# Sliding-window attention in a fused attention and mixer kernel: scores of both key tiles folded over each other in PSUM, and the turned block masked by VectorE

## The reference

```python
# 2 batches x 8 heads, seq 768, head_dim 64, n_sink 4, window 128
scores = scale * np.matmul(q, k.transpose(0, 1, 3, 2))
is_sink = pos[None, :] < int(n_sink)
rel = pos[:, None] - pos[None, :]
in_window = (rel >= 0) & (rel < int(window))
scores = np.where(is_sink | in_window, scores, -1000000000.0)
scores = scores - np.max(scores, axis=-1, keepdims=True)
a = np.exp(scores)
a = a / (np.sum(a, axis=-1, keepdims=True) + 1e-09)
return np.matmul(a, v)
```

## Time and profile before

| | us |
|---|---|
| median of 3 runs | 461.25 (458.89 to 461.72) |
| the profiled execution | 462.87 |
| its span | 461.1 |
| PE busy | 435.3 |
| DVE busy | 227.0 |
| ACT busy | 171.4 |
| POOL busy | 176.4 |

### The profile page before, as it was taken

How to read it: one execution, slowest core, us unless ns; L and a number is a source line. 1 busy time by engine, 2 the same in 40 slices (tenths; PEclk the granted TensorE clock), 3 DMA queues, 4 the chain that set the end, 5 groups by cost and what they waited for, 6 DMA issues and landing times.

```text
span 461.1 us, 7348 instructions
## 1 busy us (share of the span) xinstructions
PE 435.3 (94%) x2752; PEld 376.1 (82%) x2752; DVE 227.0 (49%) x435; ACT 171.4 (37%) x418; POOL 176.4 (38%) x122
## 2 busy tenths in 40 slices
PE   0699999999995999999999999999999999999997
PEld 0477777777774889999999997887887889999885
DVE  1568777777745799422233465615615403332222
ACT  2256665566532876322334103524323321111221
POOL 2298777543000008887765300000000165433442
PEclk9999999999997999999999999999999999999999
DMA  6444642431000002000400005000002000000222
GB/s 205 181 145 136 218 133 101 149 116 43 1 1 5 1 2 91 1 0 18 166 1 0 1 13 228 0 1 0 1 1 91 0 0 1 1 0 0 81 101 91
DMA packets 9442, 26.80 MB, mean 58 GB/s; under 512 B 1216, under 2 KB 2240, under 8 KB 9408
## 3 DMA queue, kind: packets, MB, share of 16 engines
q1 hardware_dynamic: 8064, 21.11, 13.2%
q0 software_dynamic: 1344, 5.24, 3.2%
HBM read 23.20 MB, written 3.15 MB: 57 GB/s over the span
## 4 chain that ended last, share of the span: by engine, by line
PE 92%; DVE 3%; DMA 2%; ACT 1%; issue 1%; POOL 0%; SPq 0%; ACTq 0%; DVEq 0%
PE ps L1060 22%; PE ps L1061 22%; PE ps L1062 22%; PE ps L1109 7%; PE ps L1081 6%; PE ps L1091 5%; PE ps L1075 3%; DMA lims_i<-in_window 2%; PE ps L1122 2%; PE ps L1116 2%; PE ps L1093 1%; DVE x2l L981 0%; DVE x L978 0%; ACT x2h L689 0%; POOL zl L470 0%
## 5 line engine op out<-in xcount | busy, mean ns | idle before, releaser
L527 ACT ACTIVATE probs<-ps,neg_max 128x288 f32<-128x288 f32 (+2 forms) x96 | 46.0, 495 | 52.5 <-DVE neg_max L782 52.5
L1060 PE MATMUL ps<-tok_hi,zl 128*128 128x384 f32 x192 | 64.2, 335 | 0.2 <-POOL zl L470 0.2
L1061 PE MATMUL ps<-tok_lo,zh 128*128 128x384 f32 x192 | 64.1, 334 | 0.0
L1062 PE MATMUL ps<-tok_hi,zh 128*128 128x384 f32 x192 | 64.1, 334 | 0.0
L470 POOL TENSOR_TENSOR zl<-cos_sb,zh 128x768 fp32r<-128x768 f32 x8 | 19.0, 2370 | 70.7 <-ACT zh L631 70.6
L955 DVE TENSOR_TENSOR x_t<-ps,x_t 128x768 f32<-128x768 f32 x16 | 15.3, 957 | 58.9 <-PE ps L1062 58.8
L782 DVE TENSOR_REDUCE neg_max<-ps 128x1 f32<-128x288 f32 (+2 forms) x96 | 36.3, 420 | 15.1 <-PE ps L1081 15.0
L1060 PEld LDWEIGHTS ps<-tok_hi,zl 128*128 128x128 f32 x192 | 36.0, 188 | 0.6 <-POOL zl L470 0.6
L1061 PEld LDWEIGHTS ps<-tok_lo,zh 128*128 128x128 f32 x192 | 36.0, 188 | 0.0
L1062 PEld LDWEIGHTS ps<-tok_hi,zh 128*128 128x128 f32 x192 | 36.0, 188 | 0.0
L1075 PE MATMUL ps<-bias,ident_b 128*128 128x288 bf16 (+2 forms) x96 | 19.2, 284 | 15.6 <-DVE k_lo L846 15.6
(11 more groups left out here) (142 smaller groups left out, 1064.2 us busy)
## 6 DMA issues: line engine op xcount, KB each, us to landing
tok_raw<-in_w_tok SPq DMA_DIRECT2D x6, 768.0 KB, 6.5
k_raw<-in_k_t SPq DMA_DIRECT2D x8, 448.0 KB, 4.2
q_raw<-in_q_t SPq DMA_DIRECT2D x8, 384.0 KB, 3.5
v_raw<-in_v_p SPq DMA_DIRECT2D x8, 384.0 KB, 3.0
out<-o_sb SPq DMA_DIRECT2D x12, 256.0 KB, 2.0
sp_raw<-in_w_sp SPq DMA_DIRECT2D x3, 768.0 KB, 6.3
in_raw<-in_moe_w_in POOLq DMA_DIRECT2D x1, 2048.0 KB, 8.4
th_raw<-in_moe_w_theta POOLq DMA_DIRECT2D x1, 1024.0 KB, 9.7
```

What stands on the lines that cost most here:

```text
L527: act.activation(probs[i % 2][:, 0:ncols(i), h], s_ps[i % 2][:, h, 0:ncols(i)], ACT.Exp, bias=neg_max[:, i % 2, h:h + 1], accum_out=sums[: ...
L1060: pe.matmul(dst, w_lo, m_hi, start=first, stop=False)
L1061: pe.matmul(dst, w_hi, m_lo, start=False, stop=False)
L1062: return pe.matmul(dst, w_hi, m_hi, start=False, stop=last)
```

## The change

- Keys: the layout in DRAM has the sinks behind every key tile but the last, so tile 1 also gets a product of 288 columns (tile before, sinks, own tile).
- Masks: no bias on the window parts. Instead DVE copies, under a lower triangle, the own tile's scores over those of the tile before (`copy_predicated`, both heads in one instruction, PSUM to PSUM). The folded block of 128 columns and the 32 sinks behind it are what maxima and exponentials read (160 columns). A bias remains for the sinks: two products of 32 columns on 64 rows for each head, issued behind the first part of the scores. For tile 0 the full bias remains, also behind the first part.
- Turning: one transpose for each head, and one for the sinks from tile 1 on, all in one bank, two banks in turn. DVE multiplies the turned block of both heads by two triangles into four blocks (`diagonal`, 512 elements), the factors for V of the own tile and the tile before. ACT copies the sinks' columns only, after DVE's product, as both read one bank.
- Order: on DVE `maxima(m + 2)` comes before `diagonal(m)`.
- Start: the limits are loaded by ACT's queue at once; DVE makes the triangles, then q_lo and k_lo, and only then waits for the limits and makes the three biases.
- ACT and DVE have pairs 2 to 5 written out.

```diff
-K_COLS = 2 * P + (TILES - 2) * STEP
+K_COLS = P + (TILES - 1) * STEP
+FOLD = P + SINKS
...
-        pt_ps = banks[2]
+        pt_ps = [banks[2][:, b, :] for b in range(2)]
...
             load_qk(0, 0)
-            sp.dma_start(lims_i[:, 0:2], n_sink.partition_broadcast(P)).then_inc(s_lims, 16)
-            sp.dma_start(lims_i[:, 2:4], window.partition_broadcast(P)).then_inc(s_lims, 16)
             load_v(0, 0)
...
             def copy_pt(m, i):
-                act.wait_ge(s_pt[0], m + 1)
-                act.activation(p_t[i % 2][0][:, 0:pt_cols(i, 0)], pt_ps[:, 0, 0:pt_cols(i, 0)], ACT.Copy).then_inc(s_ptc[0], 1)
+                act.wait_ge(s_pt, m + 1)
+                if i:
+                    act.wait_ge(s_ptd, diagonals(m // TILES, i))
+                cols = slice(WIN, WIN + P) if i else slice(0, WIN)
+                act.activation(p_t[i % 2][:, cols], pt_ps[i % 2][:, cols], ACT.Copy).then_inc(s_ptc, 1)
...
+            act.dma_start(lims_i[:, 0:2], n_sink.partition_broadcast(P)).then_inc(s_lims, 16)
+            act.dma_start(lims_i[:, 2:4], window.partition_broadcast(P)).then_inc(s_lims, 16)
             act.wait_ge(s_qk, 32)
             act.activation(q_hi[0][:, :], q_raw[:, :], ACT.Copy, scale=SCALE).then_inc(s_first, 1)
...
-            with act.Fori(1, PAIRS - 1) as n:
+            for n in range(1, PAIRS - 1):
...
+            dve.tensor_scalar(tri_r[:, :], col[:, :], line[:, 0:1], None, ALU.is_le).then_inc(s_mask, 1)
+            dve.tensor_scalar(tri_c[:, 1, :], col[:, :], line[:, 0:1], None, ALU.is_ge).then_inc(s_mask, 1)
+            dve.tensor_scalar(tri_c[:, 0, :], col[:, :], line[:, 0:1], None, ALU.is_lt).then_inc(s_mask, 1)
...
+            dve.wait_ge(s_first, 2)
+            dve.scalar_tensor_tensor(q_lo[0][:, :], q_raw[:, :], SCALE, q_hi[0][:, :].bitcast(F32), ALU.mult,
+                                     ALU.subtract).then_inc(s_first, 1)
+            dve.tensor_tensor(k_lo[0][:, :], k_raw[:, :], k_hi[0][:, :].bitcast(F32), ALU.subtract).then_inc(s_first, 1)
 
             dve.wait_ge(s_lims, 32)
...
             def maxima(m, i):
+                cols = slice(0, P)
+                if i:
+                    dve.wait_ge(s_sc, 2 * m + 2)
+                    dve.copy_predicated(s_ps[i % 2][:, :, 0:P], tri_r[:, :].bitcast(I32).unsqueeze(1).broadcast_to([P, 2, P]),
+                                        s_ps[i % 2][:, :, FOLD:FOLD + P]).then_inc(s_fold, 1)
+                    dve.wait_ge(s_fold, diagonals(m // TILES, i))
+                    cols = slice(0, FOLD)
                 for h in range(2):
                     dve.wait_ge(s_sc, 2 * m + h + 1)
-                    dve.tensor_reduce(neg_max[:, i % 2, h:h + 1], s_ps[i % 2][:, h, 0:ncols(i)], AX.X, ALU.max,
+                    dve.tensor_reduce(neg_max[:, i % 2, h:h + 1], s_ps[i % 2][:, h, cols], AX.X, ALU.max,
                                       negate=True).then_inc(s_max, 1)
+
+            def diagonal(m, i):
+                dve.wait_ge(s_pt, m + 1)
+                dve.tensor_tensor(p_d[i % 2][:, :, :, :],
+                                  pt_ps[i % 2][:, 0:2 * P].rearrange("p (h q) -> p h q", h=2).unsqueeze(1).broadcast_to([P, 2, 2, P]),
+                                  tri_c[:, :, :].unsqueeze(2).broadcast_to([P, 2, 2, P]), ALU.mult).then_inc(s_ptd, 1)
...
                 for i in range(TILES):
-                    copy_pt(m + i, i)
                     if i < TILES - 2:
                         maxima(m + i + 2, i + 2)
                     elif not last:
                         maxima(m + i + 2, i + 2 - TILES)
+                    if i:
+                        diagonal(m + i, i)
...
-                for h in range(2):
-                    pe.matmul(s_ps[i % 2][:, h, 0:ncols(i)], ident_b[:, :], BIAS[i][:, :], start=True, stop=False)
-
-                for q_part, k_part in ((q_lo[b], k_hi[b]), (q_hi[b], k_lo[b]), (q_hi[b], k_hi[b])):
+                for part, (q_part, k_part) in enumerate(((q_lo[b], k_hi[b]), (q_hi[b], k_lo[b]), (q_hi[b], k_hi[b]))):
                     for h in range(2):
                         rows = slice(h * HD, (h + 1) * HD)
...
+                        mm = pe.matmul(s_ps[i % 2][:, h, 0:keys.stop - keys.start], q_part[rows, tile], k_part[rows, keys],
+                                       start=(part == 0), stop=(part == 2))
...
+                        if part == 0 and i == 0:
+                            pe.matmul(s_ps[0][:, h, 0:P], ident_b[:, :], bias_0[:, :], start=False, stop=False)
+                        elif part == 0:
+                            pe.matmul(s_ps[i % 2][:, h, P:FOLD], (bias_1 if i == 1 else bias_2)[rows, :],
+                                      ident_b[rows, h * HD:h * HD + SINKS], start=False, stop=False)
 
             def turn_probs(m, i):
+                if m >= 2:
+                    pe.wait_ge(s_ptc, m - 1)
+                    pe.wait_ge(s_ptd, diagonals((m - 2) // TILES, (m - 2) % TILES))
                 for h in range(2):
                     pe.wait_ge(s_exp, 2 * m + h + 1)
-                    wait_later(pe, s_ptc[h], m)
-                    for _, c, dst in blocks(i):
-                        mm = pe.transpose(pt_ps[:, h, dst:dst + P], probs[i % 2][:, c:c + P, h], ident[:, :])
+                    mm = pe.transpose(pt_ps[i % 2][:, h * P:(h + 1) * P], probs[i % 2][:, 0:P, h], ident[:, :])
...
+                if i:
+                    pe.wait_ge(s_ptd, diagonals(no, i))
+                    parts = [(v_raw[b][:, i - 1 + j, :], [p_d[i % 2][:, j, h, :] for h in range(2)]) for j in range(2)]
+                    parts.append((v_sink[b][:, :], [p_t[i % 2][:, WIN:WIN + P]] * 2))
+                else:
+                    parts = [(v_raw[b][:, 0, :], [p_t[0][:, h * P:(h + 1) * P] for h in range(2)])]
```

More of the change, by code:

```diff
@@ L228, in attn_moe_gmlp @@
         s_exp = sem("exp_done")
-        s_pt = [sem(f"pt_written{h}") for h in range(2)]
-        s_ptc = [sem(f"pt_copied{h}") for h in range(2)]
+        s_pt = sem("pt_written")
+        s_ptc = sem("pt_copied")
+        s_fold = sem("scores_folded")
+        s_ptd = sem("pt_diagonal_made")
         s_pv = sem("pv_done")
@@ L315, in attn_moe_gmlp, with diagonals @@
         block = ctx.enter_context(nc.Block())
[L317 to L333, removed]
+        def diagonals(no, i):
+            return (TILES - 1) * no + i
         def z_of(turn):
@@ L850, in _ @@
             pair(0, 1, False, False)
-            with dve.Fori(1, PAIRS - 1) as n:
+            for n in range(1, PAIRS - 1):
                 for b in range(2):
@@ L1078, in scores @@
                     for h in range(2):
                         rows = slice(h * HD, (h + 1) * HD)
-                        last = q_part is q_hi[b] and k_part is k_hi[b]
-                        mm = pe.matmul(s_ps[i % 2][:, h, 0:ncols(i)], q_part[rows, tile], k_part[rows, keys], start=False,
-                                       stop=last)
-                        if last:
+                        mm = pe.matmul(s_ps[i % 2][:, h, 0:keys.stop - keys.start], q_part[rows, tile], k_part[rows, keys],
+                                       start=(part == 0), stop=(part == 2))
@@ L1084, in scores @@
+                        if part == 2:
                             mm.then_inc(s_sc, 1)
+                    for h in range(2):
+                        rows = slice(h * HD, (h + 1) * HD)
+                        if part == 0 and i == 0:
[3 more added lines that the diff above has]
+                                      ident_b[rows, h * HD:h * HD + SINKS], start=False, stop=False)
@@ L1099, in times_v @@
                 wait_later(pe, s_oc, 2 * no + i // HALVES)
[L1100 to L1101 removed]
+                pe.wait_ge(s_ptc, m + 1)
                 cols = slice(i % HALVES * P, i % HALVES * P + P)
[L1103 to L1105 removed]
+                if i:
+                    pe.wait_ge(s_ptd, diagonals(no, i))
[3 more added lines that the diff above has]
+                    parts = [(v_raw[b][:, 0, :], [p_t[0][:, h * P:(h + 1) * P] for h in range(2)])]
                 for j, (values, turned) in enumerate(parts):
@@ L1217, in _ @@
             pe.wait_ge(s_xt, 2 * BATCH * PAIRS)
-            for h in range(2):
-                pe.wait_ge(s_ptc[h], 2 * PAIRS * TILES)
+            pe.wait_ge(s_ptc, 2 * PAIRS * TILES)
+            pe.wait_ge(s_ptd, diagonals(2 * PAIRS, 0))
             for t in range(2, GT):
@@ L1325 @@
     q_t, k_all = (np.ascontiguousarray(a.transpose(0, 1, 2, 4, 3)).reshape(BATCH, PAIRS, P, SEQ) for a in (q, k))
-    pieces = [k_all[..., 0:WIN]]
-    for t in range(2, TILES):
+    pieces = [k_all[..., 0:P]]
+    for t in range(1, TILES):
         pieces += [k_all[..., 0:SINKS], k_all[..., t * P:(t + 1) * P]]
```

117 lines of the change are left out of this document (53 added, 64 removed).

## The result

| | us |
|---|---|
| changed kernel, median of 4 runs | 470.18 (468.07 to 473.02) |
| kernel before, run beside it | 460.5 (458.89 to 461.72) |
| ratio | 1.0225 [1.0185, 1.0264] |
| changed, profiled execution | 469.44, span 467.6 |

The change made the kernel 2.2% slower. I had predicted 451.4, with 0.05 for slower. Against the profiled execution of before the time rose by 6.6 us, where my sum had it fall by 9.9: 16.5 us to explain. Executions have a second, slower state; all ratios here are of fast ones alone, while the medians also count the one slow execution of e1 (462.2) and of e13 (472.2).

What follows compares the result with a forecast made beforehand. PE's work was taken to bound attention, and the late limits the start: start -4.7, attention -5.6, pipeline fill +0.4, sum -9.9 us, from 462.87 profiled to 453.0, as median 451.4; range 446 to 457.

Steps and rivals of the forecast that it cites:

- The new wait: In attention, PE held by ACT's copies behind DVE's masked product: 0.19 us at tile 1, 0.2 at the turn of o.
- N: The moment at which PE starts the V products behind the scores of tile i+2.
- the walk: Step-by-step timing of a pair's six steps across DVE, ACT and PE: +0.4 us of stalls, 13.5 us a pair.
- PE work: Transposes, bias, scores and V products of a pair: 1.15 us less, so PE alone needs 13.12 us.
- Fold, maxima, masked product: DVE's operations in attention: fold 0.42 us, a pair of maxima 0.56, masked product 0.70.
- Rivals 1 and 4: DVE's fold is dearer: 0.71 us, time 455.7 (chance 0.15); or 1.3 us, time 470.7 (chance 0.05).
- rival 3: Narrow bias products on PE cost as much as the wide ones: gain 3.4 us, time 453.6; chance 0.08.
- rival 4: Fold far dearer, with source and destination in PSUM: at 1.3 us, 16.1 a pair, time 470.7, slower; chance 0.05.
- The start: Before attention: q and k split ahead of the limits, PE starting at 10.9 instead of 15.64 us, -4.7.
- Rival 2: Limits land late, sharing DMA engines with q, k, v and w_theta: start -3.4, time 452.7; chance 0.12.
- 8.55 and 2.1: At the start: DVE done splitting q and k at 8.55 us, then 2.1 us of operations on the limits.
- the last pair gain 0.7: End of attention: last pair has two steps without scores, waiting for ACT anyhow; 7.5 x 0.75 us counted overall.

Runs made afterwards that it cites:

- e1: Changed kernel with DVE's masked product of tile i ahead of fold and maxima of tile i+2: 458.32 us, 0.9928 of the kernel before.
- e13: Changed kernel with 76 extra turns of the identity on PE before its first product: 468.81 us, 1.0194 of the kernel before.
- e2: Changed kernel with ACT's copy of o ahead of the sink copy and exponentials in a pair's fourth step: 461.96 us, 1.0042 of the kernel before.
- e5: Changed kernel with masked product before maxima, early copy of o and the limits' loads back on SP: 453.86 us, 0.9878 of the kernel before.
- e4: Changed kernel with the two limit loads back on SP's queue, between k and V: 466.31 us, 1.0133 of the kernel before.
- e3: Kernel before with the change's start alone (limits on ACT's queue, q_lo and k_lo before the limits): 464.27 us, ratio 1.0084.
- e10: Kernel before with the change's start alone and POOL's split of w_theta in four pieces: 460.9 us, ratio 1.0011.
- e7: Changed kernel with den made by scalar_tensor_tensor instead of tensor_scalar: 469.02 us, 1.0213 of the kernel before.
- e9: Changed kernel with 46 extra turns of the identity on PE before its first product: 468.31 us, 1.0166 of the kernel before.
- e16: Changed kernel with the old start (limits on SP between k and V, q_lo and k_lo behind the masks): 469.65 us, 1.0169 of the kernel before.

## Why the prediction was wrong

**The new wait: the step that failed.** Its times were right. From N = 87.17 on, the walk had ACT's copy of the sinks' columns at N+1.78 (1.85 measured), the copy of o there at N+3.2 (3.26), and PE wanting V products at N+2.07 (2.27). But I took the copy of o to matter at the turn of o alone, where PE asks at N+3.05, and wrote 0.2. The V products of tile 3 overwrite the PSUM bank that this copy reads, and wait for it (`wait_later(pe, s_oc, ...)` in `times_v`). Before, PE started them at 86.64, just behind the copy's end at 86.45 (85.97 + 0.48), so the wait didn't show: there was at most 0.2 us of slack and not the 0.9 that I read off the turn of o. My own N+3.2 less N+2.07 is 1.1, and 1.09 was measured. With 0.3 at tile 1 (0.19 predicted) the stalls are 1.4 to 1.5 a pair in place of 0.4, which with PE's 13.4 makes 14.89. From the first turn to the 14th lie 6.5 pairs: +4.7 came where -4.9 was due, 9.6 of the 16.5 us. e1 and e2 show that the order made it.

**PE work: nearly right.** 13.12 predicted; pairs without stalls take 13.36 (e5). The narrow bias pair costs 0.03 in the chain, not 0.11, but six scores beside it 0.73, not 0.60: together 0.76 where I had 0.71.

```profile
86.53 0.33 PE ps L1085 x2
86.86 0.03 PE ps L1094 x2
86.89 0.40 PE ps L1085 x4
```

The figure that I worked out from the Trainium skill (TensorE: Matmul & The Clock Gate, Back-to-back issue gap), an estimate of 0.05 for the pair, was the nearer one for the pair alone. The time that it promised was taken back by the scores beside it.

**Fold, maxima, masked product: right.** Rivals 1 and 4 fell with that, and rival 3 with the 0.03 of the bias pair. Slower came, but not by the mechanism of rival 4.

**The start: wrong twice.** First the size: -3.1 and not -4.7. Rival 2 looked at whether the limits land late; they had landed, and k was late instead (e4 gives 10.80 back). The rule of the Trainium skill (Trainium Kernel Development and Optimization, Key Constraints) that all queues share the DMA engines, which I cited for that rival, applies to k, q and V as well. My terms for the new start, 8.55 and 2.1, also add up to 10.65 and not to 10.9. Then the gain itself is gone by the first turn of o: 4.4 us of the 16.5 against my sum, which carried the gain to the end and had no term for the clock. In the changed kernel's trace TensorE runs that stretch at the lower level and stays there for longer than before; at the upper level (e13) the turn comes 4.7 us earlier. In the start alone (e3, e10) the hold of `den` behind POOL does it. I had costed POOL by its own lateness, not by what it holds on DVE.

What sets the moment at which the level rises stays open. How early PE begins does not set it: V products take 0.66 us from 23.5 on in e4, which begins first (10.80), and from 25.4 and 25.3 on in e1 and e2, which begin as late as the changed kernel (12.72, 12.82), but still 1.12 at 28.9 there, and 1.07 at 31.8 in e5 (11.21). Each of these is one execution.

**The join.** From the 14th turn to the end it cost 1.8 us more than before, where I had the last pair gain 0.7: 2.5 of the 16.5. The granted clock falls twice here, and once before:

```profile
135.00:139.00 4.00, 3.79 (x30) 3.11 (x30) 1.48 (x3) 0.80 (x3) 0.00 (x0) 0.57 0.01 2
139.00:149.00 10.00, 8.13 (x51) 5.98 (x47) 2.82 (x7) 1.81 (x4) 0.00 (x0) 1.00 0.02 4
149.00:156.00 7.00, 4.29 (x10) 3.46 (x11) 4.16 (x8) 2.64 (x6) 0.00 (x0) 0.51 0.02 6
```

How much of it is the clock and how much the waits was not separated. Most of it goes with the order: from the 14th turn of o to the 16th, 18.52 us here, it is 15.6 in e1, 16.0 in e2 and 15.1 in e5, under the 16.15 of before. With the order of the change it is 17.0 in e4, e7 and e9 and 18.5 in e13 and e16, so about 1.5 us of it come and go between executions. What wasn't tried is an accumulator bank for each half of o, since all banks are in use. Whether unrolled loops cost anything stayed open.

## What to carry to other kernels

When an instruction on one engine gets later, list everybody who waits for its semaphore, writers of the buffer that it reads among them, and compute the slack at the first of them; a wait that is satisfied just in time leaves no trace in a profile. Before paying with a reordering for shorter work, check which of two instructions on the helping engine the bottleneck needs first. An earlier start is worth only what arrives at the end: check what its new position coincides with on the other engines, and at which clock the gained stretch runs.

## What the runs showed of the hardware

- A VectorE operation on 128x6 elements, 0.16 us by itself, took up to 4.06 us (e1) beside one long GpSimd instruction on SBUF; each one that took over 0.9 us ended within 0.05 us of such an instruction's end. With that instruction in pieces of 1.28 us it took 0.28 at that place, and still 1.75 later in the same run (e10, at 62.03), beside a GpSimd instruction of 1.82.
- copy_predicated from PSUM to PSUM, 256 elements: 0.43 us, the price of a plain copy.
- With two 1 KB loads issued on ACT's queue beside q and k on SP's, and V 0.9 us earlier behind those, k landed 1.7 us later (q_hi at 6.68 against 4.97).
- TensorE leaves the lower level (V products of 1.12 us, and 0.66 at the upper) at very different times in kernels whose first products start 0.4 us apart: by 23.5 us in e4 (10.80), and not before 31.8 in e5 (11.21). The granted clock in the profile reads 1.00 from 12.5 to 30 us of the changed kernel, where these products took 1.12.
